# Attention scores of nine units on three PSUM banks in rotation, with VectorE taking the next unit's first maximum before this unit's second head's reciprocals

## The reference, cut to what matters

```python
# attention: q, k, v are (2 batches, 8 heads, 576, 64)
scores = scale * np.matmul(q, k.transpose(0, 1, 3, 2))
mask_local = (rel >= 0) & (rel < 32)                       # heads 0 to 3
mask_strided = (rel >= 0) & (pos[None, :] % 32 == pos[:, None] % 32)   # heads 4 to 7
scores = np.where(masks[None, :, :, :], scores, -1000000000.0)
scores = scores - np.max(scores, axis=-1, keepdims=True)
attn = np.exp(scores)
attn = attn / (np.sum(attn, axis=-1, keepdims=True) + 1e-09)
return np.matmul(attn, v)
# x (1152 rows x 512) -> dense MoE over 8 experts (w1 512x1024, ReLU, w2 1024x512) -> top-2 MoE
```

## Time and profile before

| | |
|---|---|
| median of three runs | 1188.2 us (1187.76 to 1194.41) |
| the profiled execution | 1194.28 us |
| its span | 1192.5 us |
| TensorE busy in the span | 1165.0 us (98%) |
| VectorE, ScalarE, GpSimd busy | 486.9, 325.2, 106.7 us |
| share of TensorE in the chain that ended last | 95% |

### The profile page before, as it was taken

The page is one execution under the profiler, slowest core; times in us unless marked ns, Lnnn a source line. Parts: engine busy times, 40 slices in busy tenths (PEclk is TensorE's granted clock), DMA queues, the critical chain, the costliest instruction groups (busy, mean ns, idle before and its releaser), DMA issues.

```text
span 1192.5 us, 19152 instructions
## 1 busy us (share of the span) xinstructions
PE 1165.0 (98%) x6697; PEld 1036.7 (87%) x6697; DVE 486.9 (41%) x1003; ACT 325.2 (27%) x710; POOL 106.7 (9%) x118
## 2 busy tenths in 40 slices
PE   7999999999999999999999999999997999999997
PEld 4677999999999999999999999999896889888885
DVE  4656524213323322411322332241136566665663
ACT  4763113102112211301211221231132334343332
POOL 3222000000000000000000000000001222222221
PEclk9689999999999999999999999999998999999999
DMA  7635104002201200400220220040003666556653
GB/s 167 153 111 163 50 1 137 5 0 70 70 0 57 84 0 0 141 0 0 70 70 0 69 72 0 0 142 27 27 18 103 183 187 178 160 155 166 164 154 79
DMA packets 82337, 96.42 MB, mean 81 GB/s; under 512 B 22176, under 2 KB 56992, under 8 KB 82304
## 3 DMA queue, kind: packets, MB, share of 16 engines
q1 hardware_dynamic: 76400, 81.23, 22.7%
q0 software_dynamic: 5904, 14.75, 5.8%
HBM read 85.05 MB, written 10.91 MB: 80 GB/s over the span
## 4 chain that ended last, share of the span: by engine, by line
PE 95%; DVE 1%; ACT 1%; issue 1%; SPq 1%; DMA 1%; POOL 0%; POOLq 0%; ACTq 0%; DVEq 0%
PE bank L1151 15%; PE bank L1137 15%; PE bank L1153 15%; PE bank L1152 15%; PE bank L1139 14%; PE bank L1138 14%; PE bank L1069 1%; PE bank L1082 1%; PE bank L1358 1%; ACT prs L570 1%; PE bank L1280 1%; PE bank L1060 1%; PE bank L1046 1%; PE bank L1343 1%; PE bank L1185 0%
## 5 line engine op out<-in xcount | busy, mean ns | idle before, releaser
L1151 PE MATMUL bank<-w2hi,hhi 128*128 128x512 f32 (+1 forms) x768 | 301.0, 392 | 0.0
L1153 PE MATMUL bank<-w2hi,hlo 128*128 128x512 f32 (+1 forms) x768 | 299.9, 390 | 0.0
L1152 PE MATMUL bank<-w2lo,hhi 128*128 128x512 f32 (+1 forms) x768 | 299.7, 390 | 0.0
L1137 PE MATMUL bank<-xhi,w1hi 128*128 (+1 forms) x768 | 257.9, 336 | 2.9 <-issue 2.6
L647 ACT ACTIVATE hhi<-bank 128x384 fp32r<-128x384 f32 x184 | 90.5, 492 | 611.8 <-PE bank L1139 611.8
L1139 PE MATMUL bank<-xhi,w1lo 128*128 (+1 forms) x768 | 257.0, 335 | 0.0
L1138 PE MATMUL bank<-xlo,w1hi 128*128 (+1 forms) x768 | 256.8, 334 | 0.0
L745 DVE SCALAR_TENSOR_TENSOR hlo<-bank,hhi 128x384 fp32r<-128x384 f32 (+1 forms) x256 | 139.0, 543 | 265.7 <-ACT hhi L647 234.3
L1153 PEld LDWEIGHTS bank<-w2hi,hlo 128*128 128x128 f32 (+1 forms) x768 | 141.6, 184 | 33.1
L1152 PEld LDWEIGHTS bank<-w2lo,hhi 128*128 128x128 f32 (+1 forms) x768 | 141.7, 184 | 31.0
L1151 PEld LDWEIGHTS bank<-w2hi,hhi 128*128 128x128 f32 (+1 forms) x768 | 141.7, 185 | 30.9
(11 more groups left out here) (176 smaller groups left out, 852.1 us busy)
## 6 DMA issues: line engine op xcount, KB each, us to landing
w1raw<-in_moe_w_dram SPq DMA_DIRECT2D x68, 512.0 KB, 4.6
w2raw<-in_moe_w_dram SPq DMA_DIRECT2D x68, 512.0 KB, 4.3
qkraw<-in_q_dram SPq DMA_DIRECT2D x16, 144.0 KB
qkraw<-in_k_dram SPq DMA_DIRECT2D x16, 144.0 KB
out_dram<-ysb POOLq DMA_DIRECT2D x3, 768.0 KB, 6.4
x1rows<-acc SPq DMA_DIRECT2D x9, 256.0 KB, 2.0
vloc<-in_v_dram SPq DMA_DIRECT2D x8, 144.0 KB
vstr<-in_v_dram SPq DMA_DIRECT2D x8, 144.0 KB
```

The costliest lines, as they stand in the source:

```text
L1137: pe.matmul(bank[:, 0:n], wh, xh(c), start=(c == 0), stop=False)
L1151: pe.matmul(psY[tt][0:rows, :], hh, w2hi[:, f, :], start=(f == 0), stop=False)
L1152: pe.matmul(psY[tt][0:rows, :], hh, w2lo[:, f, :], start=False, stop=False)
L1153: ins = pe.matmul(psY[tt][0:rows, :], hl, w2hi[:, f, :], start=False, stop=(f == FC - 1))
```

## The change

Three things are changed, for the units below `ROUND` = `FILL` - 1 = 9.

1. The scores of unit U, head h, go to bank (0, 1, 4)[(2U + h) % 3]. So the first head's bank was last used by the second head of unit U-2, and the second head's by the first head of unit U-1, and the mask matmuls wait for those exponentials. The mask matmuls stand ahead of the waits for the queries and keys of the pair. `keep_warm` writes the bank that the next unit's first head will use. `nmax` has a row for each parity of the unit.
2. VectorE takes the maximum of unit U+1, head 0, in the step of unit U, ahead of the reciprocals of unit U, head 1. Unit U+1's step then holds only the second head's maximum.
3. The copies of the next pair's keys stand ahead of the reciprocals of both heads; they stood behind those of the first.

```diff
+        ROUND = FILL - 1
+        def psS(U, h):
+            return (banks[0], banks[1], banks[4])[(2 * U + h) % 3 if U < ROUND else h]
+        def exps_before(U, h):
+            return max((2 * V + j + 1 for V in range(U) for j in range(2) if psS(V, j) is psS(U, h)), default=0)
...
             for U in range(UNITS):
                 rows, tiles, w = unit_shape(U)
-                for h in range(2):
-                    dve.wait_ge(scores_ready, 2 * U + h + 1)
-                    if U:
-                        dve.wait_ge(exp_ready, 2 * (U - 1) + h + 1)
-                    dve.tensor_reduce(nmax[0:rows, h, 0:tiles], by(psS[h][0:rows], w, tiles * w), AX.X, ALU.max,
-                                      negate=True).then_inc(max_ready, 1)
+                if not 0 < U < ROUND:
+                    maxima(U, 0)
+                maxima(U, 1)
...
                 if U:
                     probs_T(U - 1)
+                if U % 2 == 1 and U // 2 + 1 < ALLPAIRS:
+                    keys(U // 2 + 1, 0)
+                    keys(U // 2 + 1, 1)
                 for h in range(2):
+                    if h == 1 and U + 1 < ROUND:
+                        maxima(U + 1, 0)
                     dve.wait_ge(exp_ready, 2 * U + h + 1)
...
-                pe.wait_ge(qT_act, g + 1)
...
                 for h in range(2):
-                    if U:
-                        pe.wait_ge(exp_ready, 2 * (U - 1) + h + 1)
-                    pe.matmul(by(psS[h][0:rows], w, tiles * w), identb[0:rows, 0:rows], m, start=True, stop=False)
+                    if exps_before(U, h):
+                        pe.wait_ge(exp_ready, exps_before(U, h))
+                    pe.matmul(by(psS(U, h)[0:rows], w, tiles * w), identb[0:rows, 0:rows], m, start=True, stop=False)
+                pe.wait_ge(qT_act, g + 1)
...
-                if WARM_FROM <= U < FILL - 1:
-                    keep_warm(WARM_LOCAL if g % PAIRS < LOCAL_PAIRS else WARM_STRIDED)
+                if WARM_FROM <= U < ROUND:
+                    pe.wait_ge(exp_ready, exps_before(U + 1, 0))
+                    keep_warm(WARM_LOCAL if g % PAIRS < LOCAL_PAIRS else WARM_STRIDED, psS(U + 1, 0))
...
                 if U == FILL - 1:
                     pe.wait_ge(xlo_ready, UNITS // 2)
+                    pe.wait_ge(exp_ready, 2 * ROUND)
```

More of the change, by code:

```diff
@@ L159, in moe_stack_kernel @@
         pT = over("pT", [P, 2, HALF], F32)
-        nmax = over("nmax", [QT, 2, 4], F32)
+        nmax = over("nmax", [QT, 2, 2, 4], F32)
         rsum = over("rsum", [QT, 2, 4], F32)
@@ L570, in exps @@
                     ins = act.activation(prs[0:rows, U % 2, h, t * w:(t + 1) * w],
-                                         psS[h][0:rows, t * w:(t + 1) * w], ACT.Exp,
-                                         bias=nmax[0:rows, h, t:t + 1], accum_out=rsum[0:rows, h, t:t + 1])
+                                         psS(U, h)[0:rows, t * w:(t + 1) * w], ACT.Exp,
+                                         bias=nmax[0:rows, U % 2, h, t:t + 1], accum_out=rsum[0:rows, h, t:t + 1])
                 ins.then_inc(exp_ready, 1)
@@ L753, in sum_parts, with maxima @@
                                   ).then_inc(lg_copied, 1)
+            def maxima(U, h):
+                rows, tiles, w = unit_shape(U)
+                dve.wait_ge(scores_ready, 2 * U + h + 1)
+                if U >= 2:
+                    dve.wait_ge(exp_ready, 2 * (U - 2) + h + 1)
+                dve.tensor_reduce(nmax[0:rows, U % 2, h, 0:tiles], by(psS(U, h)[0:rows], w, tiles * w), AX.X, ALU.max,
+                                  negate=True).then_inc(max_ready, 1)
             queries(0)
@@ L809, in _ @@
             dve.wait_ge(lgT_summed, 3)
[L810 removed]
+            dve.tensor_copy(lgT1[:, LT:], banks[1][0:2 * E, 0:LT]).then_inc(lgT_dve, 1)
             split_w2(3)
@@ L1052, in scores @@
                 rows, tiles, w = unit_shape(U)
+                m = mask_l[:, half, :, :] if c < LOCAL_PAIRS else spread(mask_s[:, :], 1, 4)
+                for h in range(2):
+                    if exps_before(U, h):
+                        pe.wait_ge(exp_ready, exps_before(U, h))
+                    pe.matmul(by(psS(U, h)[0:rows], w, tiles * w), identb[0:rows, 0:rows], m, start=True, stop=False)
                 pe.wait_ge(qT_act, g + 1)
@@ L1055, in scores @@
                 pe.wait_ge(kT_ready, 2 * g + 2)
-                m = mask_l[:, half, :, :] if c < LOCAL_PAIRS else spread(mask_s[:, :], 1, 4)
-                for h in range(2):
-                    if U:
-                        pe.wait_ge(exp_ready, 2 * (U - 1) + h + 1)
-                    pe.matmul(by(psS[h][0:rows], w, tiles * w), identb[0:rows, 0:rows], m, start=True, stop=False)
                 for t in range(tiles):
@@ L1068, in scores @@
                             key = STRIDE + query
-                        ins = pe.matmul(psS[h][0:rows, t * w:(t + 1) * w],
+                        ins = pe.matmul(psS(U, h)[0:rows, t * w:(t + 1) * w],
                                         qT[g % 2][h * DH:(h + 1) * DH, query:query + rows],
@@ L1181, in group2, with keep_warm @@
                         behind[tt]()
-            def keep_warm(count):
+            def keep_warm(count, bank):
                 for i in range(count):
-                    pe.matmul(psF[0][:, :], warm[:, 0:P], warm[:, :], start=True, stop=True)
+                    pe.matmul(bank[:, :], warm[:, 0:P], warm[:, :], start=True, stop=True)
             def fill(f):
@@ L1191, in _ @@
             pe.wait_ge(warm_ready, 1)
-            keep_warm(WARM_START)
+            keep_warm(WARM_START, banks[0])
             pe.wait_ge(ident_ready, 1)
@@ L1195, in _ @@
                 if n == 1:
-                    keep_warm(WARM_FIRST)
+                    keep_warm(WARM_FIRST, banks[0])
                 for half in range(2):
@@ L1216, in _ @@
                 if U == 0:
-                    keep_warm(WARM_FIRST)
-                if WARM_FROM <= U < FILL - 1:
-                    keep_warm(WARM_LOCAL if g % PAIRS < LOCAL_PAIRS else WARM_STRIDED)
+                    keep_warm(WARM_FIRST, psS(1, 0))
+                if WARM_FROM <= U < ROUND:
+                    pe.wait_ge(exp_ready, exps_before(U + 1, 0))
+                    keep_warm(WARM_LOCAL if g % PAIRS < LOCAL_PAIRS else WARM_STRIDED, psS(U + 1, 0))
                 if U >= FILL:
@@ L1245, in _ @@
             for j in range(2):
-                logits(psS[j], WHOLE * P + j * LT, LT)
+                logits(banks[j], WHOLE * P + j * LT, LT)
             pe.wait_ge(ones_ready, 1)
```

7 lines of the change are left out of this document (2 added, 5 removed).

## The result

The changed kernel takes 1210.47 us (median of four runs, 1209.41 to 1213.26) against 1189.36 us of the kernel before (four runs). The ratio on record is 1.0147, with a 95% interval of 1.0096 to 1.0198: slower by 1.5%. The prediction was 1203.4 us with a range of 1188 to 1210, so direction and cause were as forecast, the size was too small, and the median lies 0.5 us above the end of the range. The profiled execution took 1211.45 us with a span of 1209.7 us, 17.2 us longer than before.

The account below looks back on a forecast made before the run. The prediction took TensorE, busy for 98% of the span, as the bound. The loop with half clock from about S(4) puts S(9) 9.1 us later: 1194.3 + 9.1 = 1203.4 us, range 1188 to 1210.

Parts of the forecast that it names:

- What bounds the kernel: TensorE, busy 98% of the span; a shift of the attention's end moves the kernel's end by the same amount.
- S(10): S(U) is the end of unit U's scores in the attention, read as the start of the transposes behind them.
- The moved maximum closes a loop: Attention: chain over VectorE, GpSimd and TensorE sets the unit's period, 4.85 us at full clock, 7.4 at half; before 4.26, 6.41.
- The third bank alone: Attention, units 1 to 3: removes waits for the second head's exponentials, saving at most about 1 us each.
- Where it starts: First units of the attention: S(1) stays at 16.8 us, S(2) about 21.4, S(4) at 30.8.
- The clock: Attention: TensorE's clock falls to half at about S(4), two units earlier than before, giving S(9) = 67.8, 9.1 us later.
- The upper bound of the argument: Attention: half clock from S(2) on, giving S(9) = 73.2, 14.5 us later.
- The sentence on `keep_warm`: Attention: three `keep_warm` matmuls in a strided unit did not lift the clock; nothing before the logits should.
- The Trainium skill's rule: Attention: units half at full, half at low clock, 6.1 us each, S(9) = 61.4, execution 1197 us; within the 0.20 rival.
- The relation to the median: Whole kernel: median before is 6.1 us below the profiled execution; not taken off, as most runs should have the low stretch.
- The loop, but the clock holds: Rival for the attention: loop at full clock or with a late fall, 1187 to 1196 us; chance 0.20.
- The loop does not bind: Rival for the attention: VectorE's maximum comes early enough, 1 us saved in each of units 1 to 3, 1180 to 1191; chance 0.12.

Follow-up runs that it names:

- the filled kernel: Changed kernel plus six matmuls on zeros in units 1 to 8, between the two heads' transposes where TensorE waits for GpSimd: 1193.29 us, ratio 1.001.
- the kernel with units 1 to 3 filled: Changed kernel plus six matmuls on zeros between the two heads' transposes in units 1, 2 and 3 only: 1201.67 us, ratio 1.0046.
- the kernel before with its waits filled: Kernel before plus three matmuls on zeros at the start of the steps of units 2 to 8, ahead of the masks: 1189.4 us, ratio 0.9942.

## Why the prediction was right, and where it was short

**What bounds the kernel.** Right. A later end of the attention moved the end of the kernel by the same amount: 17.1 of 17.2 us. Over all traces this holds to within 3 us, the spread of the time behind S(10).

**The moved maximum closes a loop.** Right, place and price. The chain was put at 4.86 and 4.77 us at full clock and taken as 4.85; the filled kernel took 4.94 (local to strided) and 4.91, and 4.99 on average. At half clock it was put at 7.38 and taken as 7.4; the changed kernel took 7.52 (units 5 and 6), and 7.46 on average. The gap in it was put at about 1.5 us; rows of the changed kernel have 1.49 in unit 1 and 1.01 to 1.22 at half clock. The moved maximum alone on two banks gave the whole loss.

**The third bank alone.** "At most about 1 us each" in units 1 to 3 was a bound; about 1.2 us in all came, and the times don't resolve it. The place was right, before S(5), but the cause is doubtful. The keys' copies ahead of the reciprocals were costed "at nothing", because "each wait is for something that ends before TensorE arrives". That was not so in the kernel before: masks waited 1.35 and 0.62 us for those copies (at 20.45, just ahead of the first line of rows 4, and at 29.20), more than the 0.60 and 0.92 for exponentials. At a later place the new order may also have cost something: the filled kernel's two units of 5.34 and 5.68 us. That the exponentials fill ScalarE from unit 4 on was not tested by itself.

**Where it starts.** S(1) at 16.7 was right. S(2) was put at 21.4 and came at 23.59. The 2.2 us are the half clock: from 18.66 us, where the second head's transposes began as forecast, TensorE had no gap until S(2) and took 4.93 us where 2.7 had been worked out.

**The clock.** This is the term that was mis-sized. "Between them I take the fall at about S(4)" set it at 31 us; it fell at 18.9, right behind the first gap of the loop (1.49 us at 17 to 18.7 us). The upper bound of the argument had it falling from S(2) on, 14.5 us later than before; the fall even before S(2) gives 17.1. The argument had the first gap's place and length and still kept the clock up for two more periods. Filling that gap moved the fall to 24 us, and filling three moved it to about 35. With it there, the time was 1201.67 us, where 1203.4 had been worked out. So the period was right and the fall was misplaced: the first gap's part of that is 1210.5 - 1206.9 = 3.6 us, the next two's 1206.9 - 1201.7 = 5.2. What makes the clock fall stays open. The length of a gap alone does not: "in smaller gaps" was not quite so, since the kernel before had one of 1.35 us at 19.1 to 20.45 us and its clock stayed up, while the changed one's fell behind 1.49. And the argument left out that in the profile before the clock was already at half from 12.2 to 15.5 us.

**The sentence on `keep_warm`** was wrong as a rule: "nothing before the logits should lift it". In the kernel with units 1 to 3 filled it rose at 38.3 us, and with the maximum alone on two banks at 45.2. The Trainium skill's rule ("TensorE: Matmul & The Clock Gate", A second HAM failure mode: psum-queue depth-cycling), that short idle times between groups make the clock go back and forth, had been put into a rival case because of one trace. The trace of the kernel with units 1 to 3 filled does agree with it: 0.56, 0.99, 0.50. In the changed kernel's the clock did not come back until 83.8 us.

**The relation to the median.** "The two runs at 1188 probably had a shorter one" fits, but no run near 1188 us has a trace. The 31 runs group by their clock, and the kernel before with its waits filled has only times near the lowest group (1185.4 to 1190.1 us). Where the median of so few runs lies is chance: it was 1188.2 with three runs, 1189.36 with four and 1194.79 with 31. By the last the change costs 1.3%.

**The rivals.** "The loop, but the clock holds" was built and gives 1193.29 us where 1187 to 1196 stood. "The loop does not bind" fell with every trace that has the moved maximum.

## What to carry to other kernels

An instruction that is pulled forward in an in-order queue takes its wait with it: before pulling it, follow who waits for what now stands behind it, and whether that chain comes back to the thing it waits for. If it does, the chain's length is the period, and no extra buffer shortens it. And where a trace shows TensorE's clock falling, price a new gap at both clocks and from the first unit where it appears; here the gap itself cost 4 to 7 us, by the kernel it is held against, and the clock 17. Before giving a wait to one cause, list all waits of the stretch: here the copies of the keys held TensorE longer than the exponentials that the third bank was aimed at.

## What was not expected of the hardware

- A loss of clock was bought back with matmuls that have no use: six for each unit took the time from 1210.5 to 1193.3 us.
- The kernel before falls into groups near 1187, 1195, 1200 and 1203 us with mean clocks of 0.992, 0.980, 0.973 and 0.968, and with three more such matmuls in each of seven units all ten runs lie between 1185.4 and 1190.1.
- The gap of 1.49 us in unit 1 brought the early fall: the clock fell 0.3 to 1.3 us behind its end in all three traces that have it open and in none of the three with it filled. But a gap of 1.35 us in the kernel before brought none.
- The clock can come back in the middle of such a stretch, for one unit, and fall again (38.5 to 44.8 us in the kernel with units 1 to 3 filled, about 45.2 to 48.8 us with the maximum alone on two banks).
- The same product on GpSimd took 1.49 us when it started just behind VectorE's low part of w1, and 0.66 us otherwise. Only the kernels with the keys' copies moved forward show it.
